# Attention with sinks, SoLU and routed experts on one core: the last products with v one step sooner, the next pair's first transposes one step later, and x rounded beside those transposes' copies

## The chip, the cores and the metric

The kernel runs on one core of one Trainium2 chip. The metric is the time of one execution on the device, in microseconds (us); lower is better.

## The reference

Three parts follow one another. Only the first is touched by the change.

```python
def _attn_ref(q, k, v, n_sink, window):          # 2 batches, 8 heads, 768 tokens, 64 wide
    scores = scale * np.matmul(q, k.transpose(0, 1, 3, 2))
    keep = is_sink | in_window                   # 4 sink columns, a window of 128
    scores = np.where(keep, scores, -1000000000.0)
    scores = scores - np.max(scores, axis=-1, keepdims=True)
    a = np.exp(scores)
    a = a / (np.sum(a, axis=-1, keepdims=True) + 1e-09)
    return np.matmul(a, v).astype(np.float32)

x = attn_out.transpose(0, 2, 1, 3).reshape(1536, 512)
x = _moe_ref(x)     # softmax-gated layer of 1024, layer norm, back to 512
out = _moe2_ref(x)  # 8 experts: relu(x @ w1[e]) @ w2[e], weighted by 8 rounds of row and column scaling
```

## The kernel before, in words

**Pairs and steps.** The 16 heads of the attention are worked off as 8 pairs (p = 0 to 7). The two heads of a pair lie on the upper and lower 64 rows of q, k and the output. A pair has 6 steps (t = 0 to 5), one for each tile of 128 queries; in each step there are two tiles of scores, one for each head, numbered k = 2t and 2t + 1. A tile is 128 x 128 (t = 0), 128 x 256 (t = 1) or 128 x 260 (the rest, where the four sink columns stand beside the window's 256).

**One program for each engine.** Each engine has its own list of instructions, written out by hand, and semaphores hold the lists together. In every step each engine first does the new tiles, and then calls a function `back(p, t)`, which holds the work that lags behind. The order in `back` is what the change edits, in three engines:

- TensorE: `scores(p, t + 1)` (L722), then in `back` the transposes of the probabilities (`turn(p, b)`, L742, b = 0, 1, 2 for the tiles t = 2b and 2b + 1), those of the sink columns (`turn_sinks`, L750), the products with v (`pv(p, b)`, L766), and those of the sinks (`pv_sinks`, L773), which complete the pair's x, a sum of 128 x 768 in PSUM. Most of a pair's `back` work is done while the next pair's scores are made.
- VectorE: `mask_max` (L1270, adds the mask, takes the row maximum, and empties a bank of scores; each of the two tiles of a step), then in `back` `normalise` (L1278, L1282, L1285: sum plus a small number, reciprocal, head 0's tile times it), `copy_pT` (L1291, copies head 1's transposes out of PSUM) and `rest_x` (L1303, x minus its rounded part, the low half of x).
- ScalarE: `exp_tile` (L1042, for each of the two tiles of a step), then in `back` `copy_pT` (L1049, head 0's transposes), `scale_probs` (L1057), `copy_sinkT` (L1061) and `round_x` (L1066, the rounded part of x).
- GpSimd multiplies head 1's tiles by the reciprocals (L517), splits sink columns (L540, L543), and splits the weights of the second part into a rounded and a remaining half (L556, L559, L565, L571), between these.

**What waits for what.** `rest_x(p)` waits for `round_x(p)`, and that for `pv_sinks(p)`. The first product of the next pair, `pv(p + 1, 0)`, writes into the same sum, so it waits for `rest_x(p)`. There are four banks for scores, so `scores` of a tile waits until the tile four before it has been through `mask_max`. Transposes use two banks in turn, so each waits until the use two before it has been copied. The ScalarE's `exp_tile(p, k)` waits for `mask_max(p, k)`; VectorE's `normalise(p, b)` waits for the four exponentials of its tiles.

**After the pairs** TensorE begins the second part (`h1_half`, L797 to L799) and does the last pair's remaining work between its halves.

Of the kernel before, what the change touches and what calls it, by code (L numbers as in the profile page):

```python
# [38 lines left out]
PAIRS = BATCH * HEADS // 2  # L39
# [21 lines left out]
def solu_moe(nc: bass.Bass, n_sink, window, qT, kT, v, w_in, w_out, g_ln, w_gate, w_exp, out):  # L61
# [5 lines left out]
    with ExitStack() as ctx:  # L67
# [75 lines left out]
        def x1(part, c, at, n):  # L143

            half, at = divmod(at, SEQ)
            at += half * 2 * HALF_X + part * HALF_X + c * SEQ
            return xw[:, at:at + n]
# [137 lines left out]
        def tile_probs(p, t, h):  # L285
            at = h * PW + k_from(t, h)
            return probs[:, p % 2, t, at:at + width(t)]
# [14 lines left out]
        def t_use(b, h):  # L302
            return 2 * b + h

        def t_bank(p, use):
            return bank(T_BANK + (T_USES * p + use) % 2)
# [5 lines left out]
        def copied(p, use):  # L312

            if use in ACT_USES:
                return pT_act, len(ACT_USES) * p + ACT_USES.index(use) + 1
            return pT_dve, len(DVE_USES) * p + DVE_USES.index(use) + 1

        def x_psum(t0, t1):
            return ps[:, XP + t0 * P:XP + t1 * P]
# [382 lines left out]
        def _(pe):  # L702
# [29 lines left out]
            def turn(p, b):  # L732

                for h in range(2):
                    use = t_use(b, h)
                    pe.wait_ge(probs_ready[h], BATCHES * p + b + 1)
                    if h == 0:
                        pe.wait_ge(probs_scaled, BATCHES * p + b + 1)
                    bank_free(p, use)
                    for n in range(T_FIRST[b], T_END[b]):  # L740
                        at = (n - T_FIRST[b]) * P
                        last = pe.transpose(t_bank(p, use)[:, at:at + P], p_block(p, h, n), ident[:, :])  # L742
                    last.then_inc(pT_full, 1)

            def turn_sinks(p):

                pe.wait_ge(sinks_split, p + 1)
                bank_free(p, SINK_USE)
                for t in range(2, QT):
                    last = pe.transpose(t_bank(p, SINK_USE)[0:SINK_ROWS, (t - 2) * P:(t - 1) * P],  # L750
                                        sink_cols[:, t - 2, :].bitcast(F32), ident[:, :])
                last.then_inc(pT_full, 1)

            def pv(p, b):

                for h in range(2):
                    pe.wait_ge(*copied(p, t_use(b, h)))
                if b == 0:
                    pe.wait_ge(v_loaded[p % 2], 128 * (p // 2 + 1))
                    if p > 0:  # L760
                        pe.wait_ge(x_out, p)
                for j, t0, t1 in (((0, 0, 2), (1, 1, 2)), ((1, 2, 3), (2, 2, 4)),
                                  ((3, 3, 5), (4, 4, 6), (5, 5, 6)))[b]:
                    n = j + t0
                    for h in range(2):
                        pe.matmul(x_psum(t0, t1)[64 * h:64 * h + 64, :], v_sb[:, p % 2, h, j * DH:(j + 1) * DH],  # L766
                                  pT[:, h, n * P:(n + t1 - t0) * P],
                                  start=(j, t0) in ((0, 0), (1, 2)), stop=False, skip_group_check=True)

            def pv_sinks(p):  # L770
                pe.wait_ge(*copied(p, SINK_USE))
                pe.wait_ge(v_sinks_split, p + 1)
                pe.matmul(x_psum(2, QT), v_sink_r[:, p % 2, :], sinkT[:, :],  # L773
                          start=False, stop=True, skip_group_check=True).then_inc(x_full, 1)

            def back(p, t):

                if t == 0 and p > 0:
                    turn(p - 1, 1)
                if t == 1 and p > 0:  # L780
                    pv(p - 1, 0)
                if t == 2 and p > 0:
                    turn(p - 1, 2)
                if t == 3 and p > 0:
                    turn_sinks(p - 1)
                    pv(p - 1, 1)
                if t == 4:
                    if p == 0:
                        pe.wait_ge(consts, 3)
                    turn(p, 0)  # L790
                if t == 5 and p > 0:
                    pv(p - 1, 2)
                    pv_sinks(p - 1)

            def three(o, ws, xs, first, last):

# [24 lines left out]
            for p in range(PAIRS):  # L821
                for t in range(QT):
# [4 lines left out]
                    back(p, t)  # L827
            h1_half(0, 0)
            back(PAIRS, 0)
            h1_half(0, 1)  # L830
            back(PAIRS, 1)
# [1 line left out]
            back(PAIRS, 2)  # L833
            h1_half(1, 1)
            back(PAIRS, 3)
            back(PAIRS, 5)


            def turn_ln(b, f):
# [195 lines left out]
        def _(act):  # L1035
# [9 lines left out]
            def copy_pT(p, b, h):  # L1045
                use = t_use(b, h)
                n0, n1 = T_FIRST[b], T_END[b]
                act.wait_ge(pT_full, T_USES * p + use + 1)
                act.activation(pT[:, h, n0 * P:n1 * P], t_bank(p, use)[:, 0:(n1 - n0) * P],  # L1049
                               ACT.Copy).then_inc(pT_act, 1)  # L1050

            def scale_probs(p, b):

                act.wait_ge(norm_link, 2 * (BATCHES * p + b + 1))
                a = tile_probs(p, 2 * b + 1, 0)
                k = 4 * b + 2
                act.activation(a, a, ACT.Copy, scale=a_stat[:, A_INV, k:k + 1]).then_inc(probs_scaled, 1)  # L1057

            def copy_sinkT(p):
                act.wait_ge(pT_full, T_USES * p + SINK_USE + 1)  # L1060
                act.activation(sinkT[:, :], t_bank(p, SINK_USE)[0:SINK_ROWS, 0:(QT - 2) * P],  # L1061
                               ACT.Copy).then_inc(pT_act, 1)

            def round_x(p):
                act.wait_ge(x_full, p + 1)
                act.activation(x1(0, p % DC, p // DC * SEQ, SEQ), x_psum(0, QT), ACT.Copy).then_inc(x_hi_out, 1)  # L1066

            def back(p, t):

                if t == 0 and p > 1:  # L1070
                    round_x(p - 2)
                if t == 0 and p > 0:
                    copy_pT(p - 1, 1, 0)
                    scale_probs(p - 1, 2)
                if t == 2:
                    if p > 0:
                        copy_pT(p - 1, 2, 0)
                    scale_probs(p, 0)
                if t == 3 and p > 0:
                    copy_sinkT(p - 1)  # L1080
                if t == 4:
                    copy_pT(p, 0, 0)
                    scale_probs(p, 1)

            for p in range(PAIRS):
                for t in range(QT):
# [175 lines left out]
        def _(dve):  # L1262
# [11 lines left out]
            def normalise(p, b):  # L1274

                s = slice(4 * b, 4 * b + 4)
                dve.wait_ge(exp_done, STEPS * p + 4 * b + 4)
                dve.tensor_scalar(a_stat[:, A_DEN, s], a_stat[:, A_SUM, s], EPS, None,  # L1278
                                  ALU.add).then_inc(norm_link, 1)
                n = 2 * (BATCHES * p + b)  # L1280
                dve.wait_ge(norm_link, n + 1)
                dve.reciprocal(a_stat[:, A_INV, s], a_stat[:, A_DEN, s]).then_inc(norm_link, 1)  # L1282
                dve.wait_ge(norm_link, n + 2)
                a = tile_probs(p, 2 * b, 0)
                dve.tensor_scalar(a, a, a_stat[:, A_INV, 4 * b:4 * b + 1], None, ALU.mult).then_inc(probs_ready[0], 1)  # L1285

            def copy_pT(p, b, h):
                use = t_use(b, h)
                n0, n1 = T_FIRST[b], T_END[b]
                dve.wait_ge(pT_full, T_USES * p + use + 1)  # L1290
                dve.tensor_copy(pT[:, h, n0 * P:n1 * P],  # L1291
                                t_bank(p, use)[:, 0:(n1 - n0) * P]).then_inc(pT_dve, 1)
# [7 lines left out]
            def rest_x(p):  # L1300
                dve.wait_ge(x_hi_out, p + 1)
                c, at = p % DC, p // DC * SEQ
                dve.tensor_tensor(x1(1, c, at, SEQ), x_psum(0, QT), x1(0, c, at, SEQ).bitcast(F32),  # L1303
                                  ALU.subtract).then_inc(x_out, 1)

            def back(p, t):

                if t == 0 and p > 0:
                    normalise(p - 1, 2)
                    if p > 1:  # L1310
                        rest_x(p - 2)
                    copy_pT(p - 1, 1, 1)
                if t == 2:
                    normalise(p, 0)
                    if p > 0:
                        copy_pT(p - 1, 2, 1)
                if t == 3 and p > 0:
                    rest_v_sinks(p - 1)
                if t == 4:
                    normalise(p, 1)  # L1320
                    copy_pT(p, 0, 1)


# [280 lines left out]
```

## Time and profile before

| | |
|---|---|
| median of three runs | 1254.23 us (1253.05 to 1255.44) |
| the profiled execution's own time | 1253.09 us |
| its span, first to last instruction | 1251.3 us |
| granted TensorE clock | 1.00 of full speed throughout |
| busy over the span | TensorE 99%, VectorE 55%, ScalarE 29%, GpSimd 43% |
| attention, up to the first product of the second part | the first 93.9 us |

The shares are means over stages with different limits. From 100 us on TensorE has no gaps; the attention is the only stage where it is not always busy. In the profile's rows L12 is a line of the kernel; "[0.62 <-DVE xw L1303]" behind an instruction says that its engine stood idle for 0.62 us before it, and that the wait was ended by VectorE's instruction of line 1303. PE is TensorE, DVE is VectorE, ACT is ScalarE, POOL is GpSimd.

### The profile page before, as it was taken

What the parts mean: (1) busy time and instruction counts of PE and PEld (TensorE: products, weight loads), DVE (VectorE), ACT (ScalarE), POOL (GpSimd) and SP (SyncE); (2) the same over time, 40 slices, a digit from 0 to 9 for tenths busy, and PEclk for the clock granted to TensorE, in tenths of its full rate; (3) what the DMA queues carried; (4) which work ended last, traced back from release to release, by engine and by line L of the source; (5) the groups of instructions that cost most, each with busy time, mean ns of one, the idle gap of its engine ahead of it and who ended that gap; (6) DMA issues with size and microseconds to landing.
All of it is one profiled execution on the core that took longest, in us unless ns stands there. A gap on an engine that the chain in (4) does not pass through costs nothing.

```text
span 1251.3 us, 18785 instructions
## 1 busy us (share of the span) xinstructions
PE 1236.2 (99%) x6446; PEld 1097.3 (88%) x6446; DVE 691.7 (55%) x1348; ACT 365.1 (29%) x832; POOL 535.7 (43%) x625
## 2 busy tenths in 40 slices
PE   7999999999999999999999999999999999999998
PEld 4558899989988999999999999999999999999997
DVE  7895734356665555555555555555555555555554
ACT  7884634312233222222222222222222222222221
POOL 7772315644444444444444444444444444444440
PEclk9999999999999999999999999999999999999999
DMA  6440000111110111111111111111111111111102
GB/s 204 156 149 18 1 1 1 34 35 34 34 35 28 38 36 36 34 34 34 34 34 34 34 34 34 34 34 34 34 34 34 34 34 34 34 34 34 35 18 101
DMA packets 57264, 53.13 MB, mean 42 GB/s; under 512 B 4352, under 2 KB 44544, under 8 KB 57216
## 3 DMA queue, kind: packets, MB, share of 16 engines
q1 hardware_dynamic: 56928, 52.19, 13.1%
q8 instruction: 27, 0.44, 0.1%
q10 hardware_dynamic: 288, 0.33, 0.1%
q14 instruction: 21, 0.17, 0.0%
HBM read 49.35 MB, written 3.15 MB: 42 GB/s over the span
## 4 chain that ended last, share of the span: by engine, by line
PE 95%; ACT 2%; DVE 2%; DMA 1%; issue 1%; SPq 0%; DVEq 0%; ACTq 0%
PE ps L797 30%; PE ps L798 30%; PE ps L799 30%; PE ps L722 2%; PE ps L766 1%; PE ps L742 1%; PE ps L847 1%; ACT probs L1042 1%; ACT acc L1218 1%; DVE probs L1270 1%; DMA k_sb<-kT 0%; PE ps L977 0%; DVE xw L1303 0%; ACT xw L1066 0%; DMA q_sb<-qT 0%
## 5 line engine op out<-in xcount | busy, mean ns | idle before, releaser
L1528 DVE SCALAR_TENSOR_TENSOR acc<-ps,gate_now,acc 128x512 f32<-128x512 f32 x336 | 252.1, 750 | 166.2 <-PE ps L799 162.0
L797 PE MATMUL ps<-ring 128*128 128x512 f32 x768 | 300.6, 391 | 0.0
L798 PE MATMUL ps<-ring 128*128 128x512 f32 x768 | 299.8, 390 | 0.0
L799 PE MATMUL ps<-ring 128*128 128x512 f32 x768 | 299.2, 390 | 0.0
L1200 ACT ACTIVATE sums<-ps 128x384 f32<-128x384 f32 x192 | 94.4, 492 | 597.8 <-PE ps L799 597.8
L1504 DVE TENSOR_TENSOR sums<-ps,sums 128x384 f32<-128x384 f32 x192 | 106.9, 557 | 158.2 <-ACT sums L1200 106.9
L799 PEld LDWEIGHTS ps<-ring 128*128 128x128 f32 x768 | 144.3, 188 | 30.9
L797 PEld LDWEIGHTS ps<-ring 128*128 128x128 f32 x768 | 144.2, 188 | 27.9 <-DVE acc L1524 0.4
L798 PEld LDWEIGHTS ps<-ring 128*128 128x128 f32 x768 | 144.2, 188 | 25.8
L642 POOL TENSOR_TENSOR w_raw<-w_raw 128x256 f32<-128x256 f32 x32 | 23.7, 741 | 321.3 <-PE ps L799 321.3
L797 PE MATMUL ps<-xw,ring 128*128 128x384 f32 x448 | 152.5, 340 | 0.3 <-ACT sums L1200 0.2
L1510 DVE SCALAR_TENSOR_TENSOR ring<-sums,ring 128x384 fp32r<-128x384 f32 x192 | 112.0, 583 | 72.9 <-ACT ring L1211 72.9
L799 PE MATMUL ps<-xw,ring 128*128 128x384 f32 x448 | 151.0, 337 | 0.0
L798 PE MATMUL ps<-xw,ring 128*128 128x384 f32 x448 | 150.9, 337 | 0.0
L797 PE MATMUL ps<-xw,w_b 128*128 128x384 f32 x448 | 150.5, 336 | 0.0
L799 PE MATMUL ps<-xw,w_b 128*128 128x384 f32 x448 | 150.3, 336 | 0.0
L798 PE MATMUL ps<-xw,w_b 128*128 128x384 f32 x448 | 150.0, 335 | 0.0
L671 POOL TENSOR_SCALAR ring<-w_in 128x1024 fp32r<-128x1024 f32 x32 | 33.8, 1056 | 233.0 <-PE ps L799 178.2
L1211 ACT ACTIVATE ring<-sums 128x384 fp32r<-128x384 f32 x192 | 100.1, 521 | 85.7 <-DVE sums L1504 85.7
L797 PEld LDWEIGHTS ps<-xw,ring 128*128 128x128 f32 x448 | 84.1, 188 | 2.6 <-ACT sums L1200 0.5
L798 PEld LDWEIGHTS ps<-xw,w_b 128*128 128x128 f32 x448 | 84.3, 188 | 2.0
L797 PEld LDWEIGHTS ps<-xw,w_b 128*128 128x128 f32 x448 | 84.1, 188 | 1.9
(148 smaller groups left out, 1765.2 us busy)
## 6 DMA issues: line engine op xcount, KB each, us to landing
w_in<-w_exp SPq DMA_DIRECT2D x64, 256.0 KB, 3.2
w_raw<-w_exp SPq DMA_DIRECT2D x64, 128.0 KB, 2.8
w_raw<-w_exp SPq DMA_DIRECT2D x32, 256.0 KB, 3.2
v_sb<-v SPq DMA_DIRECT2D x16, 192.0 KB
out<-acc SPq DMA_DIRECT2D x12, 256.0 KB, 2.0
q_sb<-qT SPq DMA_DIRECT2D x7, 384.0 KB, 4.4
k_sb<-kT SPq DMA_DIRECT2D x7, 384.0 KB, 4.9
k_sb<-kT SPq DMA_DIRECT2D x9, 256.0 KB, 5.7
```

What stands on the lines that cost most here:

```text
L642: pool.tensor_tensor(raw(4), raw(0), raw(3), ALU.add).then_inc(w1_sums, 1)
L671: pool.tensor_scalar(w2c(0, 0, 2 * BANK), w2_raw(0, 2 * BANK), 1.0, 0.0, ALU.mult, ALU.add).then_inc(w2_hi, 1)
L722: pe.matmul(bank(k % S_BANKS)[:, 0:w], q_sb[rows_h, p % 2, t * P:(t + 1) * P], k_sb[rows_h, p % 2, k_at(t), at:at + w], start=True, stop=T ...
L742: last = pe.transpose(t_bank(p, use)[:, at:at + P], p_block(p, h, n), ident[:, :])
L797: pe.matmul(o, ws[0], xs[0], start=first, stop=False, skip_group_check=True)
L798: pe.matmul(o, ws[0], xs[1], start=False, stop=False, skip_group_check=True)
L799: return pe.matmul(o, ws[1], xs[0], start=False, stop=last, skip_group_check=True)
L1200: act.activation(part_sum(m, s), a_bank(s), ACT.Copy).then_inc(part_copied, 1)
L1211: act.activation(h_at(0, i, b * BLK, BLK), a_bank(s) if m == C12 else c_sum(m), ACT.Relu).then_inc(h_hi_out, 1)
L1504: dve.tensor_tensor(c_sum(m), at, part_sum(part, s), ALU.add).then_inc(c_summed, 1)
L1510: dve.scalar_tensor_tensor(out=h_at(1, i, b * BLK, BLK), in0=a_bank(s) if m == C12 else c_sum(m), scalar=0.0, in1=h_at(0, i, b * BLK, BLK) ...
L1528: dve.scalar_tensor_tensor(out=acc[:, T, :], in0=y_bank(u, T), scalar=gate_now[:, T:T + 1], in1=acc[:, T, :], op0=ALU.mult, op1=ALU.add).t ...
```

## The change

In the steps t = 4 and t = 5 of a pair p, some lagging work changes places. On TensorE the last products of pair p - 1 with v and those of its sinks move from step 5 to step 4, and the first transposes of pair p from step 4 to step 5. The two copies of these transposes (ScalarE's and VectorE's) move from step 4 to step 5 too. `round_x` and `rest_x` of pair p - 1 move from step 0 of pair p + 1 to step 5 of pair p, and stand in front of these copies. After the last pair, TensorE's last call becomes `back(PAIRS, 4)`, which does what `back(PAIRS, 5)` did. Nothing is added and nothing is removed.

```diff
@@ TensorE, back(p, t)
-                if t == 4:
+                if t == 4 and p > 0:
+                    pv(p - 1, 2)
+                    pv_sinks(p - 1)
+                if t == 5:
                     if p == 0:
                         pe.wait_ge(consts, 3)
                     turn(p, 0)
-                if t == 5 and p > 0:
-                    pv(p - 1, 2)
-                    pv_sinks(p - 1)
@@ TensorE, after the pairs
-            back(PAIRS, 5)
+            back(PAIRS, 4)
@@ ScalarE, back(p, t)
-                if t == 0 and p > 1:
-                    round_x(p - 2)
                 if t == 0 and p > 0:
                     copy_pT(p - 1, 1, 0)
                     scale_probs(p - 1, 2)
...
                 if t == 4:
+                    scale_probs(p, 1)
+                if t == 5:
+                    if p > 0:
+                        round_x(p - 1)
                     copy_pT(p, 0, 0)
-                    scale_probs(p, 1)
@@ VectorE, back(p, t)
                 if t == 0 and p > 0:
                     normalise(p - 1, 2)
-                    if p > 1:
-                        rest_x(p - 2)
                     copy_pT(p - 1, 1, 1)
...
                 if t == 4:
                     normalise(p, 1)
+                if t == 5:
+                    if p > 0:
+                        rest_x(p - 1)
                     copy_pT(p, 0, 1)
```

On VectorE, from the two tiles of step 5 of a middle pair to the first tile of step 1 of the next, this stands in a row before (the `ISA` rows are `mask_max`, each with a second small row that reads its maximum; the last one here is the first tile of step 1):

```order
219 L1291 COPY pT<-ps 128x384 [waits pT_full]
220 L1270 ISA probs,a_stat<-ps,mask 128x260 [waits scores_full]
222 L1270 ISA probs,a_stat<-ps,mask 128x260 [waits scores_full]
224 L1270 ISA probs,a_stat<-ps,mask 128x128 [waits scores_full]
226 L1270 ISA probs,a_stat<-ps,mask 128x128 [waits scores_full]
228 L1278 TENSOR_SCALAR a_stat<-a_stat 128x4 [waits exp_done]
229 L1282 RECIPROCAL a_stat<-a_stat 128x4 [waits norm_link]
230 L1285 TENSOR_SCALAR probs<-probs,a_stat 128x260 [waits norm_link]
231 L1303 TENSOR_TENSOR xw<-ps,xw 128x768 [waits x_hi_out]
232 L1291 COPY pT<-ps 128x512 [waits pT_full]
233 L1270 ISA probs,a_stat<-ps,mask 128x256 [waits scores_full]
```

And this is the same stretch of the changed kernel, whose lines in this part are numbered one higher:

```order
219 L1271 ISA probs,a_stat<-ps,mask 128x260 [waits scores_full]
221 L1271 ISA probs,a_stat<-ps,mask 128x260 [waits scores_full]
223 L1304 TENSOR_TENSOR xw<-ps,xw 128x768 [waits x_hi_out]
224 L1292 COPY pT<-ps 128x384 [waits pT_full]
225 L1271 ISA probs,a_stat<-ps,mask 128x128 [waits scores_full]
227 L1271 ISA probs,a_stat<-ps,mask 128x128 [waits scores_full]
229 L1279 TENSOR_SCALAR a_stat<-a_stat 128x4 [waits exp_done]
230 L1283 RECIPROCAL a_stat<-a_stat 128x4 [waits norm_link]
231 L1286 TENSOR_SCALAR probs<-probs,a_stat 128x260 [waits norm_link]
232 L1292 COPY pT<-ps 128x512 [waits pT_full]
233 L1271 ISA probs,a_stat<-ps,mask 128x256 [waits scores_full]
```

The subtraction for x (128x768) has moved from behind the normalising to just behind the two tiles of step 5, and the copy of 384 columns from before these tiles to behind the subtraction.

On ScalarE, from step 4 of a middle pair to step 0 of the next, before (each `x2` is the two exponentials of a step):

```order
79 L1042 ACTIVATE probs,a_stat<-probs,a_stat 128x260 [waits scores_read] x2
80 L1049 ACTIVATE pT<-ps 128x384 [waits pT_full]
81 L1057 ACTIVATE probs<-probs,a_stat 128x260 [waits norm_link]
82 L1042 ACTIVATE probs,a_stat<-probs,a_stat 128x260 [waits scores_read] x2
83 L1042 ACTIVATE probs,a_stat<-probs,a_stat 128x128 [waits scores_read] x2
84 L1066 ACTIVATE xw<-ps 128x768 [waits x_full]
85 L1049 ACTIVATE pT<-ps 128x512 [waits pT_full]
```

The same stretch of the changed kernel:

```order
79 L1042 ACTIVATE probs,a_stat<-probs,a_stat 128x260 [waits scores_read] x2
80 L1057 ACTIVATE probs<-probs,a_stat 128x260 [waits norm_link]
81 L1042 ACTIVATE probs,a_stat<-probs,a_stat 128x260 [waits scores_read] x2
82 L1066 ACTIVATE xw<-ps 128x768 [waits x_full]
83 L1049 ACTIVATE pT<-ps 128x384 [waits pT_full]
84 L1042 ACTIVATE probs,a_stat<-probs,a_stat 128x128 [waits scores_read] x2
85 L1049 ACTIVATE pT<-ps 128x512 [waits pT_full]
```

The rounding of x now stands behind two exponentials of step 5, where it stood behind these and two more of step 0.

## Rows read from the trace of the kernel before

**Rows 1.** Busy time by stretch: three pairs, each from `mask_max(p, 2)` to the next, and a later stretch. Columns: length, then busy us (instructions) of PE, PEld, DVE, ACT, POOL, then clock, DMA.

```profile
28.35:40.24 11.89, 10.75 (x83) 6.82 (x81) 10.65 (x39) 10.09 (x34) 8.77 (x19) 1.00 0.56 182
40.24:51.62 11.38, 10.76 (x83) 6.76 (x81) 10.08 (x39) 9.75 (x32) 8.46 (x17) 1.00 0.54 173
...
63.01:74.74 11.73, 10.76 (x83) 6.76 (x81) 10.71 (x39) 9.87 (x32) 8.50 (x17) 1.00 0.52 182
...
100.00:150.00 50.00, 50.00 (x260) 40.67 (x259) 30.98 (x61) 25.91 (x45) 13.67 (x21) 1.00 0.00 1
```

**Rows 2.** Who waited for whom, 20 to 112 us: total us, times, longest.

```profile
PE ps L766 <- DVE xw L1303: 4.0, 5, 1.1
...
DVE xw L1303 <- ACT xw L1066: 1.4, 5, 0.5
```

**Rows 3.** The chain that ended last, one pair's turn: start us, us, what.

```profile
58.93 1.87 ACT probs L1042 x8
60.80 0.70 ACT xw L1066
61.53 0.97 DVE xw L1303
```

**Rows 4.** Timeline of DVE between two pairs: start us, us, instruction, idle before.

```profile
58.01 0.54 DVE L1291 COPY pT<-ps 128x384 f32<-128x384 f32 x1
58.48 0.41 DVE L1270 CUSTOM_DVE_ANT_0 probs<-ps,mask 128x260 f32<-128x260 f32 x1
...
59.17 0.28 DVE L1270 CUSTOM_DVE_ANT_0 probs<-ps,mask 128x128 f32<-128x128 f32 x1
...
60.06 0.17 DVE L1278 TENSOR_SCALAR a_stat<-a_stat 128x4 f32<-128x4 f32 x1 [0.40 <-ACT probs L1042]
...
61.53 0.96 DVE L1303 TENSOR_TENSOR xw<-ps,xw 128x768 fp32r<-128x768 f32 x1 [0.23 <-ACT xw L1066]
62.41 0.68 DVE L1291 COPY pT<-ps 128x512 f32<-128x512 f32 x1
63.01 0.41 DVE L1270 CUSTOM_DVE_ANT_0 probs<-ps,mask 128x256 f32<-128x256 f32 x1
```

**Rows 5.** Timeline of ACT in the same place.

```profile
59.44 0.50 ACT L1042 ACTIVATE probs<-probs,a_stat 128x260 f32<-128x260 f32 x1
...
59.94 0.39 ACT L1042 ACTIVATE probs<-probs,a_stat 128x128 f32<-128x128 f32 x1
...
60.70 0.80 ACT L1066 ACTIVATE xw<-ps 128x768 fp32r<-128x768 f32 x1
```

**Rows 6.** Timeline of PE around the moved work.

```profile
56.76 0.87 PE L742 MATMUL ps<-ident,probs 128*128 128x128 f32 x6
57.57 0.49 PE L722 MATMUL ps<-k_sb,q_sb 64*128 64x128 f32 x4
...
59.22 0.50 PE L773 MATMUL ps<-sinkT,v_sink_r 72*128 72x512 f32 x1
...
62.64 0.87 PE L766 MATMUL ps<-pT,v_sb 128*64 128x256 f32 x8 [0.62 <-DVE xw L1303]
```

**Rows 7.** Timelines of the second pair's end: PE at the load of q and k, DVE, POOL.

```profile
23.72 0.49 PE L722 MATMUL ps<-k_sb,q_sb 64*128 64x128 f32 x4 [1.27 <-DMA k_sb<-kT]
...
24.84 1.06 DVE L1278 TENSOR_SCALAR a_stat<-a_stat 128x4 f32<-128x4 f32 x1
...
24.59 1.28 POOL L571 TENSOR_TENSOR w_end<-w_raw,w_end 128x512 fp32r<-128x512 f32 x1
```

**Rows 8.** Timelines: one DVE operation of three pairs, and POOL's beside the longest.

```profile
20.14 0.28 DVE L1297 TENSOR_TENSOR v_sink_r<-v_sink,v_sink_r 8x128 fp32r<-8x128 f32 x1
...
55.62 0.50 DVE L1297 TENSOR_TENSOR v_sink_r<-v_sink,v_sink_r 8x128 fp32r<-8x128 f32 x1
...
67.00 0.86 DVE L1297 TENSOR_TENSOR v_sink_r<-v_sink,v_sink_r 8x128 fp32r<-8x128 f32 x1
...
66.45 1.27 POOL L565 TENSOR_TENSOR xw<-w_raw,xw 128x512 fp32r<-128x512 f32 x1
```

## The prediction, made before the changed kernel was run

> **What bounds the kernel now.** I read the busy times by stretch first. From 100 us on TensorE is busy for the whole of the stretch [rows 1]; the change touches nothing there, so a microsecond won or lost before it is one at the end. In the attention a pair takes 11.38 us (one in the middle 11.73, the first full one 11.89), with TensorE busy for 10.76, VectorE for 10.08 and ScalarE for 9.75 [rows 1]. No engine is full, and three are nearly so: a loop through several engines sets the pace. The list of waits names it: TensorE's first products with v wait for VectorE's subtraction for x (`rest_x`), 4.0 us in 5 times, and that one for ScalarE's rounding (`round_x`), 1.4 us in 5 times [rows 2]. The chain of waits goes through the same place in each pair: four exponentials, `round_x`, `rest_x` [rows 3], and then the product with v [rows 6].
>
> The reader is to see in VectorE's timeline how little room it has there. From the first tile of step 5 (58.48) to the first tile of step 1 (63.01) are 4.53 us, and it stands idle in them for only 0.40 (for the exponentials) and 0.23 (for `round_x`) [rows 4]. So its own work there is 4.53 - 0.63 = 3.90 us. TensorE waits 0.62 us in the same place [rows 6], as does ScalarE elsewhere: both follow VectorE.
>
> **The change part by part.** Nothing is added, so everything is a matter of who stands where.
>
> *TensorE.* Six transposes (0.81 us from start to start of what follows, 56.76 to 57.57) go behind the twelve products and the sinks' one; x of a pair is then complete one `turn` and one `scores` sooner. Before, the sinks' product starts at 59.22 [rows 6]; without the transposes (0.81) and the scores of the next pair's first tiles (0.4 of their 0.49, since instructions overlap) ahead of it, it starts near 58.0 and x is complete near 58.5. That is before ScalarE can come to it, as the next part shows, so x itself is never what is late.
>
> *ScalarE.* `round_x` now stands behind the two exponentials of step 5. The first starts 0.45 us behind its tile's `mask_max` (58.48 to 58.93), the second 0.51 later (59.44), and what follows 0.50 after that (59.94) [rows 3 to 5]: `round_x` can start 0.45 + 0.51 + 0.50 = 1.46 us after the first tile of step 5. Before, it stood two exponentials of step 0 later, at 60.70, which is 2.22 after.
>
> *VectorE.* `rest_x` starts 0.83 us after `round_x` starts (60.70 to 61.53) [rows 4, 5]: so 1.46 + 0.83 = 2.29 us after the first tile. But VectorE, which formerly had two more tiles and the normalising to do in between, now comes to it right after its two tiles, 0.69 us after the first one (58.48 to 59.17), with a last read of about 0.1. It stands idle for 2.29 - 0.69 - 0.1 = 1.5 us, in every pair. What it gets back: the 0.40 it waited for the exponentials (they are done long before, now) and the 0.23 for `round_x`. The copy of 384 columns (0.47, 58.01 to 58.48) moves from one side of this to the other: the stretch has it more, the rest of the pair has it less.
>
> Sum for a pair: +1.50 - 0.40 - 0.23 = **+0.87 us**. The stretch of 4.53 becomes 3.90 + 0.47 + 1.50 = 5.87, the rest of the pair (11.38 - 4.53 = 6.85) becomes 6.38, together 12.25.
>
> Is the idle time hidden by anything? What is queued behind `rest_x` on VectorE is the copy of the first transposes, then the tiles of step 0 of the next pair, then the normalising that GpSimd and ScalarE wait for. TensorE's next transposes wait for that copy (the bank rule), and the scores of step 2 wait for the tiles of step 0. TensorE has 0.62 us of idle time and no more to lend, and needs its turn with VectorE again within the pair. Nothing hides it.
>
> *The ends.* It counts from pair 2 on. The scores of pair 2 are held by the load of k until 23.72 [rows 7] in both orders. Before, VectorE is then stopped in a small operation of `normalise` for 1.06 us, until GpSimd's operation beside it ends (24.59 + 1.28 = 25.87; 24.84 + 1.06 = 25.90) [rows 7], and reaches the first tile of step 1 at 28.35 [rows 1]. After, the thirteen products stand ahead of the held scores, so x is complete before 23.72. I put `round_x` at 23.4 and `rest_x` 0.83 later, near 24.2 (an estimate); then 0.88 for it, 0.47 for the copy, 0.5 for two tiles of 128 (59.17 to 60.06, less 0.40), 1.24 for the normalising (60.06 to 61.53, less 0.23) and 0.60 for a copy [rows 4] bring the first tile of step 1 to about 27.9. The small operation now comes after 25.87 and isn't stopped: a gain of 0.5 us. From there five pair turns follow before the second part begins (three of them are in [rows 1]), and each costs 0.87. The last pair's idle time lies beside the first products of the second part and costs nothing.
>
> Sum: -0.5 + 5 x 0.87 = **+3.8 us**. Against the profiled execution (1253.09 us, 1.8 more than its span) this makes 1256.9; the median of the runs is 1.1 us above that execution, so against it 1254.2 + 3.8 = **1258.0 us**, +0.3%. About 0.2%, 2.5 us, is what a measurement of this kernel can tell from no change.
>
> **A price that is not in the sum: GpSimd.** The operation of 1.06 us [rows 7] and the one of 0.86 against 0.50 in another pair (67.00 + 0.86 = 67.86, right after GpSimd's 66.45 + 1.27 = 67.72) [rows 8] show VectorE's operations on SBUF ending just after one of GpSimd's. The slower of these pairs is the one of 11.73 instead of 11.38 [rows 1], so such a stop passes into the pair's time in full. The change moves VectorE's normalising against GpSimd's row of work: `normalise(p, 2)` comes about 1.2 us nearer to `normalise(p + 1, 0)`, so GpSimd's later work is still under way when VectorE comes to its next small operations. From below a pair gains 0.22 (0.50 down to 0.28 [rows 8]); from above it loses 0.36 (0.86 against 0.50), or more if two such operations meet one of GpSimd's. I take nothing, and keep -0.2 to +0.5 a pair for the range.
>
> The Trainium skill, "SBUF — State Buffer", section "Who interferes with whom", says that VectorE and GpSimd share a pair of ports as an exclusive lock, and whichever operation comes second is blocked until the first ends. By that rule, and these rows agree (the end at 25.90 behind 25.87), the order of arrival in the new rhythm decides, and the sum would be up to 2.5 us more.
>
> **The rivals.**
>
> 1. *TensorE sets the pace, and the change frees it.* x is complete sooner, `rest_x` is over long before the next pair's first product, and the wait of 0.62 (in all 4.0 us [rows 2]) goes, with nothing in its place. For it: this wait is the longest of TensorE's, and TensorE is the busiest of the three. Time: 1254.2 - 4.0 = 1250 us. It is decided by whether VectorE can spare 1.5 us in a pair: it would need idle time elsewhere of at least 0.9 us, and outside the stretch its timeline shows only 11.38 - 10.08 - 0.63 = 0.67, most of it gaps between dependent small operations. I give it 0.09.
> 2. *The gaps are shared out.* VectorE waits the 1.5 us, but the work after it is no longer held up by other waits and stops: GpSimd's stops fall away (-0.2), other waits (0.3 or so) too. Then a pair costs 0.3 to 0.4 and the total is -0.5 + 5 x 0.35 = +1.3: 1255.5 us. 0.15.
> 3. *GpSimd's stops get worse*: up to 0.5 a pair on top, +3.8 + 2.5 = +6.3: 1260.5 us. 0.16.
> 4. The forecast, +2.6 to +5.2: 0.60.
>
> **How the numbers follow.** The time is that of case 4. It alone spans 1256.8 to 1259.4. The range for 8 in 10 takes in most of cases 2 and 3 and leaves out case 1: 1255.4 to 1260.5. Slower by over 0.2%: case 4 and case 3, 0.76; within 0.2%: case 2 and what noise takes from the others, 0.15; faster: case 1, 0.09.
>
> **What would show it.** In the changed kernel: `rest_x` with an idle time before it near 1.5 us, released by `round_x`, in pairs 2 to 7; the wait of TensorE's first products for `rest_x` gone, and in its place waits of transposes on VectorE's copy and of scores on `mask_max`; pairs of about 12.2 us from one first tile of step 1 to the next; the second part beginning near 97.5 instead of 93.9; stretches from 100 us on unchanged in length. It is wrong if ScalarE's `round_x` starts before the exponentials' row says it can, if VectorE proves to have room (pairs below 11.4), or if small operations of VectorE get long beside GpSimd's (pairs of 12.7 and more).

## The result, and the profile after

| | before | after |
|---|---|---|
| median | 1253.64 us (6 runs, 1252.11 to 1255.93) | 1258.40 us (6 runs, 1257.93 to 1260.63) |
| profiled execution, its span | 1253.09, 1251.3 us | 1258.81, 1257.0 us |
| ratio to before | | 1.0047, 95% interval 1.0037 to 1.0057 |

The changed kernel is slower by 0.47%, and the interval lies wholly above the 0.2% that count as no change. (The ratio of the two medians is 1.0038; 1.0047 is the recorded estimate from all the runs, which the interval belongs to.) The forecast was 1258.0 us, +3.8 us. The spans differ by 5.7 us, and so the forecast's sum was too small by nearly 2 us; the medians differ by 4.8.

First the busy times of the changed kernel, from one `mask_max(p, 2)` to the next as in [rows 1] (length, then busy us of PE, PEld, DVE, ACT, POOL), and a late stretch:

```profile
27.52:40.34 12.82, 11.24 (x85) 6.81 (x81) 10.92 (x40) 10.20 (x34) 8.46 (x16) 1.00 0.57 191
40.34:53.15 12.81, 10.94 (x83) 6.66 (x79) 10.91 (x40) 9.98 (x32) 8.45 (x16) 1.00 0.47 153
53.15:65.95 12.80, 10.95 (x83) 6.66 (x79) 10.90 (x40) 9.98 (x32) 8.84 (x18) 1.00 0.49 150
65.95:78.75 12.80, 10.94 (x83) 6.66 (x79) 10.90 (x39) 9.98 (x32) 8.46 (x16) 1.00 0.46 165
...
100.00:150.00 50.00, 50.00 (x261) 40.69 (x260) 29.60 (x57) 24.28 (x45) 14.25 (x25) 1.00 0.04 11
```

A pair now takes 12.81 us instead of 11.38. TensorE is still full in the late stretch, so nothing is won back there. VectorE is busy for 10.91 us in a pair instead of 10.08 with the same instructions: 0.83 us of busy time without more work.

Who waited for whom in the changed kernel, 20 to 112 us (us in total, times, longest):

```profile
DVE xw L1304 <- ACT xw L1066: 10.9, 7, 1.8
...
PE ps L742 <- ACT pT L1049: 5.3, 5, 1.1
...
PE ps L742 <- DVE pT L1292: 2.3, 5, 0.5
...
PE ps L722 <- DVE a_stat L1271: 1.7, 5, 0.3
```

Against [rows 2]: VectorE's wait for `round_x` has grown from 1.4 to 10.9 us. TensorE's wait for `rest_x` (4.0 us) is gone, and in its place it waits 9.3 us for copies of transposes and for `mask_max`. Its timeline has the three places:

```profile
50.13 0.63 PE L742 MATMUL ps<-ident,probs 128*128 128x128 f32 x4 [1.07 <-ACT pT L1049]
51.21 0.63 PE L742 MATMUL ps<-ident,probs 128*128 128x128 f32 x4 [0.45 <-DVE pT L1292]
...
53.61 1.05 PE L722 MATMUL ps<-k_sb,q_sb 64*128 64x260 f32 x4 [0.34 <-DVE a_stat L1271]
...
99.50 0.47 PE L797 MATMUL ps<-xw 128*128 128x512 f32 x1 [0.41 <-DVE a_stat L1271]
```

The last of these rows is the first product of the second part: 99.50 against 93.88 before, 5.6 us later. That is the whole difference of the spans. The chain that ended last goes through the same place, over the two exponentials and the rounding to `rest_x` (start us, us, what; [rows 3] have it before, with four exponentials where two are now; each counts twice, with its small read):

```profile
47.81 1.10 ACT probs L1042 x4
48.91 0.70 ACT xw L1066
...
49.64 0.04 DVE xw L1304
```

VectorE's timeline for the stretch of [rows 4], and on to the next first tile of step 5:

```profile
47.35 0.42 DVE L1271 CUSTOM_DVE_ANT_0 probs<-ps,mask 128x260 f32<-128x260 f32 x1
...
49.64 0.96 DVE L1304 TENSOR_TENSOR xw<-ps,xw 128x768 fp32r<-128x768 f32 x1 [1.51 <-ACT xw L1066]
50.51 0.55 DVE L1292 COPY pT<-ps 128x384 f32<-128x384 f32 x1
...
53.15 0.41 DVE L1271 CUSTOM_DVE_ANT_0 probs<-ps,mask 128x256 f32<-128x256 f32 x1
...
54.72 0.81 DVE L1279 TENSOR_SCALAR a_stat<-a_stat 128x4 f32<-128x4 f32 x1
...
57.39 0.89 DVE L1298 TENSOR_TENSOR v_sink_r<-v_sink,v_sink_r 8x128 fp32r<-8x128 f32 x1
...
60.16 0.41 DVE L1271 CUSTOM_DVE_ANT_0 probs<-ps,mask 128x260 f32<-128x260 f32 x1
```

The stretch from 47.35 to 53.15 has grown from 4.53 to 5.80 us: 0.47 for the copy that moved into it, and 0.80 of time lost. `rest_x` starts 2.29 us after the first tile, as forecast, with 1.51 us of idle time before it. The rest of the pair (53.15 to 60.16) is 7.01 us, where the forecast had 6.38. Two small operations are long in it, an addition of `normalise(p, 0)` of 0.81 us (such an addition takes 0.17 in [rows 4]) and the subtraction for the sinks' part of v (`rest_v_sinks`) of 0.89 (0.50 in [rows 8]). GpSimd's timeline beside them:

```profile
54.31 0.61 POOL L556 TENSOR_SCALAR xw<-w_raw 128x512 fp32r<-128x512 f32 x1
54.89 0.62 POOL L559 TENSOR_SCALAR w_end<-w_raw 128x512 fp32r<-128x512 f32 x1
...
56.86 1.27 POOL L565 TENSOR_TENSOR xw<-w_raw,xw 128x512 fp32r<-128x512 f32 x1
```

54.89 + 0.62 = 55.51, and VectorE's addition ends at 54.72 + 0.81 = 55.53. 56.86 + 1.27 = 58.13, and its subtraction ends at 57.39 + 0.89 = 58.28. The addition started while the first of GpSimd's two roundings ran, and was held through the second as well. In the kernel before, the same addition came when GpSimd's second rounding was all but over (52.64 + 0.61 = 53.25), and was not held; the copy behind it then waited for its transposes:

```profile
52.64 0.61 POOL L559 TENSOR_SCALAR w_end<-w_raw 128x512 fp32r<-128x512 f32 x1
...
53.21 0.17 DVE L1278 TENSOR_SCALAR a_stat<-a_stat 128x4 f32<-128x4 f32 x1
...
54.21 0.69 DVE L1291 COPY pT<-ps 128x512 f32<-128x512 f32 x1 [0.30 <-PE ps L742]
```

### The profile page after: what moved, and what is told of

The parts are those of the page before. It is cut to its first block, busy times and chain, and to the rows that moved or that the text cites. A ratio compares the mean times of both kernels' runs of the same rounds, so it can differ in the third digit from the quotient of the medians.

```text
span 1257.0 us, 18785 instructions
## 1 busy us (share of the span) xinstructions
PE 1237.0 (98%) x6446; PEld 1097.1 (87%) x6446; DVE 693.8 (55%) x1348; ACT 365.8 (29%) x832; POOL 535.7 (43%) x625
## 4 chain that ended last, share of the span: by engine, by line
PE 93%; DVE 2%; ACT 2%; issue 1%; DMA 1%; POOL 0%; SPq 0%; DVEq 0%; ACTq 0%
PE ps L797 30%; PE ps L798 30%; PE ps L799 30%; PE ps L722 1%; DVE probs L1271 1%; PE ps L742 1%; PE ps L847 1%; DMA k_sb<-kT 1%; ACT probs L1042 1%; ACT acc L1219 1%; PE ps L977 0%; DVE v_sink_r L1298 0%; DVE pT L1292 0%; ACT xw L1066 0%; PE ps L766 0%
```

## The experiments

Two questions are put. Is it the place of x's two halves that costs, by VectorE's wait for `round_x` (theory A), or TensorE's new order, by transposes that come too late to be copied (theory B)? And are GpSimd's stops a cost of their own? All kernels compute the reference's result in full. Ratios are to the kernel before, on the same chip; a pair is again the time from one `mask_max(p, 2)` to the next, read from each profile at the middle pairs.

| kernel | median us | before, same chip | ratio (95% interval) | pair us |
|---|---|---|---|---|
| changed, `rest_x` back | 1252.91 | 1253.01 | 0.9994 (0.9985 to 1.0003) | 11.63 |
| changed, both halves of x back | 1255.21 | 1253.01 | 1.0028 (1.0016 to 1.0039) | 12.01 |
| before, `round_x` early | 1252.31 | 1253.01 | 0.9993 (0.9984 to 1.0002) | 11.26 to 11.77 |
| changed, GpSimd's rounding later | 1257.43 | 1253.01 | 1.0033 (1.0021 to 1.0046) | 12.35 |
| changed, `round_x` first | 1250.92 | 1252.73 | 0.9986 (0.9977 to 0.9995) | 11.37 |
| the two above together | 1250.48 | 1252.73 | 0.9981 (0.9972 to 0.9990) | 11.25 |
| before, `round_x` early, v's subtraction later | 1248.80 | 1252.73 | 0.9968 (0.9956 to 0.9980) | 10.84 |
| changed, `round_x` first, v's subtraction later | 1250.32 | 1252.73 | 0.9980 (0.9971 to 0.9989) | 11.26 |
| before, v's subtraction later | 1251.02 | 1252.97 | 0.9987 (0.9978 to 0.9996) | 11.16 |
| changed, v's subtraction later | 1254.35 | 1252.97 | 1.0018 (1.0009 to 1.0027) | 12.20 |

### `rest_x` put back behind the normalising

```diff
@@ changed kernel, VectorE, back(p, t)
                     normalise(p - 1, 2)
+                    if p > 1:
+                        rest_x(p - 2)
                     copy_pT(p - 1, 1, 1)
...
                 if t == 5:
-                    if p > 0:
-                        rest_x(p - 1)
                     copy_pT(p, 0, 1)
```

> The changed kernel, with only the subtraction for x (rest_x) put back to where it stood, behind the normalising of step 0; round_x, the copies and TensorE's order stay as changed. Theory A (VectorE's 1.5 us of waiting for round_x sets the cost, and GpSimd's stops add to it): the wait of 1.5 us is gone, VectorE stops at most 0.35 us for TensorE's transposes instead, and a pair, 12.8 us in the changed kernel and 11.4 before, takes 11.4 to 11.8; the time is within 2.5 us of before. Theory B (the order on TensorE is what costs, since the transposes now end later than VectorE wants to copy them): VectorE waits 1 us and more for the transposes in the same place, a pair stays at 12 us or more, and the time is 3 us or more above before.

A pair fell from 12.81 to 11.63 us, and the time is that of the kernel before. That is what theory A expected. (GpSimd's two stops are gone here as well, so the 1.18 us that a pair fell by are not the wait alone.) VectorE's timeline shows that theory B names a real wait too:

```profile
60.32 0.56 DVE L1292 COPY pT<-ps 128x384 f32<-128x384 f32 x1 [0.98 <-PE ps L742]
```

From 25 to 84 us this wait is 0.89 to 0.98 us in five pairs and 0.57 in one. It was expected at 0.35 at most. With the transposes later on TensorE, VectorE comes to their copy early; that the changed kernel hides the same time under the wait for `round_x` is a reading here, and the run with `round_x` first bears it out. What is left of the change in this kernel, TensorE's new order with the early `round_x`, costs a pair 0.25 us (11.63 against 11.38), a sixth of the loss.

### Both halves of x put back

```diff
@@ changed kernel, with the edit above, ScalarE, back(p, t)
+                if t == 0 and p > 1:
+                    round_x(p - 2)
                 if t == 0 and p > 0:
                     copy_pT(p - 1, 1, 0)
...
                 if t == 5:
-                    if p > 0:
-                        round_x(p - 1)
                     copy_pT(p, 0, 0)
```

> The changed kernel with both parts of x (round_x on ScalarE, rest_x on VectorE) back in step 0; only TensorE's swap and the two copies stay as changed. Theory A: the wait of rest_x for round_x is 0.2 to 0.4 us again, a pair takes 11.4 to 11.9 us, the time is within 3 us of before. Theory B: pairs of 12 us or more, 3 us or more above before.

12.01 us a pair, just above theory A's 11.4 to 11.9 and at the edge of B's. The time does not choose between them either: the runs scatter from 1254.3 to 1260.7 us, and the excess over the kernel before is 2.2 us by the medians and 3.5 by the ratio, on either side of the 3 us. VectorE waits for the transposes and then for `round_x`, one after the other:

```profile
60.23 0.56 DVE L1292 COPY pT<-ps 128x384 f32<-128x384 f32 x1 [0.99 <-PE ps L742]
...
62.63 0.96 DVE L1304 TENSOR_TENSOR xw<-ps,xw 128x768 fp32r<-128x768 f32 x1 [0.28 <-ACT xw L1066]
```

TensorE's swap and its two copies therefore cost 0.63 us a pair, if nothing of x is moved with them. The expectation had both theories too far apart: what the swap costs depends on where x's halves stand.

### The kernel before with `round_x` at the end of step 5

```diff
@@ kernel before, ScalarE, back(p, t)
-                if t == 0 and p > 1:
-                    round_x(p - 2)
                 if t == 0 and p > 0:
                     copy_pT(p - 1, 1, 0)
...
                     copy_pT(p, 0, 0)
                     scale_probs(p, 1)
+                if t == 5 and p > 0:
+                    round_x(p - 1)
```

> The kernel before, with only round_x moved, to the end of step 5, where x has just been completed; rest_x stays behind the normalising of step 0. Theory A says that the loop exponentials, round_x, rest_x, tiles of the next pair holds the pair, and that VectorE's idle 0.23 us for round_x and TensorE's 0.62 us for rest_x can go once round_x is early: pairs of 11.0 to 11.2 instead of 11.4, the time 1 to 2 us below before. Rival: the two exponentials of step 0 come 0.7 us later and VectorE's or ScalarE's next waits take the place: no difference beyond 0.1%.

No difference that can be told. The wait of 0.23 us before `rest_x` is gone as expected, yet the pairs did not get shorter (11.72, 11.49, 11.26, 11.77 and 11.27 us). The reading is that the time went to GpSimd's stops: VectorE's small subtraction for v takes 0.71 us in one pair and 1.22 in the next, where it took 0.50 and 0.86. It is tried further down, by moving that subtraction.

```profile
55.78 0.71 DVE L1297 TENSOR_TENSOR v_sink_r<-v_sink,v_sink_r 8x128 fp32r<-8x128 f32 x1
...
61.59 0.94 DVE L1303 TENSOR_TENSOR xw<-ps,xw 128x768 fp32r<-128x768 f32 x1
...
67.05 1.22 DVE L1297 TENSOR_TENSOR v_sink_r<-v_sink,v_sink_r 8x128 fp32r<-8x128 f32 x1
```

### The changed kernel with GpSimd's rounding of weights behind the next normalising

```diff
@@ changed kernel, GpSimd
                 normalise(p, 0)
                 if p > 0:
+                    round_segments(p)
                     rest_w_in(p)
...
                 round_v_sinks(p)
-                if p + 1 < PAIRS:
-                    round_segments(p + 1)
```

> The changed kernel, with GpSimd's rounding of a pair's two pieces of weights (0.6 us each) moved behind the next pair's first normalising, so that it no longer runs while VectorE does the small addition of normalise(p, 0). If GpSimd's stop of 0.82 us of that addition is part of the cost: it takes 0.17 again, and a pair takes 0.3 to 0.4 us less than 12.8 (the rest of the 0.65 is covered by VectorE's former wait of 0.3 for the transposes), the time is 1.5 to 2.0 us below the changed kernel, some 3 us above before. If the stop is hidden elsewhere: pairs of 12.8 us and no difference to the changed kernel.

The stop is part of the cost: a pair takes 12.35 instead of 12.81. The addition takes 0.17 again, VectorE's subtraction for v 0.42, and a third small operation is now held (0.43; this kernel's lines are numbered one lower):

```profile
67.58 0.17 DVE L1278 TENSOR_SCALAR a_stat<-a_stat 128x4 f32<-128x4 f32 x1
...
68.59 0.69 DVE L1291 COPY pT<-ps 128x512 f32<-128x512 f32 x1 [0.30 <-PE ps L741]
...
70.00 0.42 DVE L1297 TENSOR_TENSOR v_sink_r<-v_sink,v_sink_r 8x128 fp32r<-8x128 f32 x1
...
71.16 0.43 DVE L1278 TENSOR_SCALAR a_stat<-a_stat 128x4 f32<-128x4 f32 x1
```

The rows add up to it: 0.25 (the copy of 128x512 starts 2.58 us after the first tile of step 1, where it started 2.83 after) + 0.47 (0.89 to 0.42) - 0.26 (0.17 to 0.43) = 0.46.

In all it gained less than five times 0.46, and less than the expectation had: the median is 4.4 us above the kernel before, where some 3 were expected, and the intervals of this run and of the changed kernel overlap. The first product of the second part starts at 98.19 instead of 99.50, since the second pair reaches its first tile of step 1 at 28.95 instead of 27.52. The cause of that lies in the trace: the moved work of GpSimd now meets VectorE's subtraction for v in the second pair, and holds it through three operations in a row (it took 0.30 us there in the changed kernel; 19.86 + 1.27 = 21.13, and 18.77 + 2.51 = 21.28).

```profile
18.77 2.51 DVE L1297 TENSOR_TENSOR v_sink_r<-v_sink,v_sink_r 8x128 fp32r<-8x128 f32 x1
...
19.86 1.27 POOL L565 TENSOR_TENSOR xw<-w_raw,xw 128x512 fp32r<-128x512 f32 x1
```

### The changed kernel with `round_x` ahead of step 5's exponentials

```diff
@@ changed kernel, ScalarE, back(p, t)
                 if t == 4:
                     scale_probs(p, 1)
+                    if p > 0:
+                        round_x(p - 1)
                 if t == 5:
-                    if p > 0:
-                        round_x(p - 1)
                     copy_pT(p, 0, 0)
```

> The changed kernel with one instruction moved on ScalarE: round_x stands ahead of step 5's two exponentials instead of behind them (x is complete some 0.6 us before ScalarE could start them). Everything else, TensorE's order and GpSimd's work with it, is as changed. Theory A (the 1.5 us that VectorE waits for round_x are the price): rest_x can start as soon as VectorE has done its two tiles, and it covers the wait for the transposes that showed (0.98 us) when rest_x was put back; the stretch from the first tile of step 5 to that of step 1 falls from 5.80 to 4.4 to 4.6 us, a pair takes 11.3 to 11.6 with GpSimd's stops as they are, and the time is 1 to 2 us below the kernel before. Rival: the exponentials, 0.7 us later, are what VectorE's next normalising waits for, and a pair stays at 12 us or more.

This is the run that decides. One instruction of ScalarE moved past two others, and the whole loss is gone: a pair takes 11.37 us, and the kernel is, if anything, faster than before (0.9986, interval up to 0.9995, which is less than the 0.2% that count as a change). VectorE's timeline:

```profile
57.12 0.96 DVE L1304 TENSOR_TENSOR xw<-ps,xw 128x768 fp32r<-128x768 f32 x1
58.00 0.55 DVE L1292 COPY pT<-ps 128x384 f32<-128x384 f32 x1
...
60.63 0.41 DVE L1271 CUSTOM_DVE_ANT_0 probs<-ps,mask 128x256 f32<-128x256 f32 x1
...
62.21 0.81 DVE L1279 TENSOR_SCALAR a_stat<-a_stat 128x4 f32<-128x4 f32 x1
...
64.87 0.89 DVE L1298 TENSOR_TENSOR v_sink_r<-v_sink,v_sink_r 8x128 fp32r<-8x128 f32 x1
```

No idle time stands before `rest_x` or the copy behind it, so `rest_x` covers the wait for the transposes. GpSimd's two stops are there in full, 0.81 and 0.89 us, as in the changed kernel. The wait of 1.51 us and the stops, which made the rest of the pair 0.63 longer, are thus separate terms, and this run takes away the first alone: 12.81 - 11.37 = 1.44.

### `round_x` first, with GpSimd's rounding later

The two edits above together.

> The kernel with round_x first and GpSimd's rounding of the weights behind the next pair's first normalising, both at once. If GpSimd's stops are a cost of their own that adds to the order of x, a pair takes 0.3 to 0.5 us less than with round_x first alone, 10.9 to 11.1, and the time is 3 us below before. If TensorE (10.4 us of work in a pair and a stagger of 0.35 in its scores) now sets the pace, no more than 0.1 us a pair is gained.

A miss: 11.25 us a pair, where 10.9 to 11.1 was expected, and no difference to `round_x` first alone that the intervals can tell. The stops are shorter (0.17, 0.42, 0.43; but in the second pair the subtraction is held for 2.50 us, as with GpSimd's rounding moved alone, and the pairs begin 2.06 us later than with `round_x` first alone). And x is now not complete in time. TensorE's sinks' product is what `round_x` waits for, and `rest_x` for it (the lines are again numbered one lower):

```profile
DVE xw L1303 <- ACT xw L1065: 2.5, 6, 0.5
ACT xw L1065 <- PE ps L772: 1.7, 6, 0.3
```

This is nearly the rival of that run, TensorE setting the pace (it is busy for 10.75 us of the pair by the trace, where the expectation took 10.4). The chain that ended last shows the loop, and neither VectorE nor GpSimd is in it from 60 to 74 us:

```profile
68.81 0.44 PE ps L772
...
69.28 0.82 ACT xw L1065
70.09 0.98 ACT probs L1041 x4
71.07 0.39 ACT pT L1048
...
71.60 1.07 PE ps L741 x8
```

From the sinks' product it goes through `round_x`, the two exponentials of step 5 and ScalarE's copy of the transposes, back to the transposes of TensorE that wait for that copy. Putting `round_x` ahead of the exponentials has taken it out of VectorE's way and left all three in TensorE's.

### `round_x` early in the kernel before, and the subtraction for v moved

```diff
@@ kernel before, with round_x at the end of step 5, VectorE, back(p, t)
-                if t == 3 and p > 0:
-                    rest_v_sinks(p - 1)
                 if t == 4:
+                    if p > 0:
+                        rest_v_sinks(p - 1)
                     normalise(p, 1)
```

> The kernel before, with round_x at the end of step 5 (as in the run that gained nothing) and VectorE's small subtraction for the sinks' v moved from step 3 to step 4, ahead of the normalising, where GpSimd was idle for 1.3 us. If GpSimd's stops of this operation (0.71 and 1.22 us instead of 0.28 in that run) took what the earlier round_x had given back, it takes 0.28 now and pairs of 10.9 to 11.1 appear, 1.5 to 2.5 us below before in all. If another loop holds the pair, it stays at 11.3 or more.

Pairs of 10.84 us (one of 10.95), the fastest kernel of the study: 0.9968 (0.9956 to 0.9980), 3.9 us below the median of before. Both are more than was expected (10.9 to 11.1, and 1.5 to 2.5 us). With the subtraction out of GpSimd's way the early `round_x` pays, which bears out the reading of the run that gained nothing. In front of the normalising GpSimd is idle, and the subtraction takes 0.28 us:

```profile
65.14 0.28 DVE L1297 TENSOR_TENSOR v_sink_r<-v_sink,v_sink_r 8x128 fp32r<-8x128 f32 x1
```

TensorE is now busy for 10.74 of a pair's 10.83 us (in the columns of [rows 1]), so waits and stops have next to nothing left to give:

```profile
60.45:71.28 10.83, 10.74 (x83) 6.75 (x80) 10.02 (x39) 9.81 (x32) 8.38 (x17) 1.00 0.58 200
```

### `round_x` first, and the subtraction for v moved

The same move in the kernel with `round_x` first.

> The kernel with round_x first, and the same move of VectorE's small subtraction for the sinks' v to step 4. It removes one of GpSimd's two stops (0.89 to 0.28 us) and leaves the other (the 0.82 us of the small addition): pairs 0.3 to 0.6 us shorter than with round_x first alone, the time 2 to 4 us below before. If stops are covered by waits, no difference to it.

A miss by size: 11.26 us a pair instead of 10.8 to 11.1. The subtraction takes 0.28, but 0.57 us of idle time before `rest_x` came back, released by `round_x`:

```profile
57.93 0.96 DVE L1304 TENSOR_TENSOR xw<-ps,xw 128x768 fp32r<-128x768 f32 x1 [0.57 <-ACT xw L1066]
```

The pair is that of `round_x` first with GpSimd's rounding later, and the chain that ended last has the same loop (55 to 70 us: sinks' product, `round_x`, exponentials, copy, transposes, without VectorE and GpSimd). That is why two different stops, each taken away from the kernel with `round_x` first, end at the same 11.25 us: in this order the loop is what is left.

### The subtraction for v moved alone, in both kernels

> The kernel before with only VectorE's small subtraction for the sinks' v moved from step 3 to step 4, ahead of the normalising; round_x stays in step 0. It tells the two moves of the fastest kernel apart (10.85 us a pair, with round_x early too; round_x alone gained nothing). If the two gains are independent, this one gives what GpSimd's stop cost, 0.22 us a pair (0.50 to 0.28) and 0.58 where it was 0.86, so pairs of 11.16 and 1.5 us less in all. If the loop through round_x holds the pair, it gives less, 0.1 or nothing, since the time won goes into VectorE's wait for round_x.

> The changed kernel with only the same move of VectorE's small subtraction. GpSimd stops it for 0.61 us in each pair of the changed kernel (0.89 instead of 0.28), and VectorE is without slack from there to the tiles of step 5: a pair falls from 12.81 to 12.2, the time by 2.5 to 3 us against the changed kernel, to about 2.5 to 3 us above before. If other waits take it up, less than half of that.

Both as expected by the pair: 11.16 us in the kernel before, and 12.20 in the changed one. So in the fastest kernel, taken in this order, 0.22 us a pair are GpSimd's stop and 0.32 the early `round_x`, which gained nothing by itself. In the changed kernel the stop of the subtraction cost the full 0.61 us. There the whole time fell to 1.4 us above before, where 2.5 to 3 were expected, and by more than five times 0.61, because the second pair ended 0.75 us sooner as well (first tile of step 1 at 26.77 instead of 27.52).

## Why the prediction was right, point by point

**The place was right.** The forecast said that VectorE would stand idle 2.29 - 0.69 - 0.1 = 1.5 us before `rest_x`; it is 1.51, and `rest_x` starts 2.29 us after the first tile of step 5. The stretch was to be 5.87 us and is 5.80. That this wait costs what it seems to is shown by the run with `round_x` first, where it alone is taken away, and a pair falls by 1.44.

**What hides nothing.** TensorE's waits moved from `rest_x` to VectorE's copy and `mask_max`, as forecast. The largest went to ScalarE's copy (1.07 us), which stands behind `round_x` too and which the forecast did not name.

**The term that was mis-sized is GpSimd's.** The forecast took nothing for it and kept -0.2 to +0.5 a pair. It measured +0.63, outside that range: the rest of the pair is 7.01 us against 6.38 forecast. By the rows, the addition's stop costs 0.24: it takes 0.64 longer, but VectorE's wait of 0.30 for the transposes behind it, which the run with GpSimd's rounding later shows again, is gone (and 0.1 of gaps), and the copy starts 2.83 us after the first tile of step 1 instead of 2.59. The subtraction's costs 0.37: the next tile starts 0.91 us after it, where it started 0.54 after. The step that failed is "I take nothing". One of the prediction's own signs of being wrong came with it, small operations of VectorE that get long beside GpSimd's and "pairs of 12.7 and more": the pairs are 12.81 us, where 12.25 were forecast. The trace of before had the material, though not the rows that the prediction showed: GpSimd's second rounding of 0.61 us ends just behind the start of the addition there, and as the normalising of one pair comes 1.2 us nearer to that of the next, it lies across the addition.

**The ends.** The gain in the second pair was put at 0.5 and is 0.83 (28.35 to 27.52). The second part was to begin near 97.5 us and began at 99.50. Its first product waits 0.41 us for the last `mask_max`, which the forecast did not have. Of the five turns two were longer before than the 11.38 that was reckoned with, 11.89 and 11.73 [rows 1], and all are near 12.8 now. From the first tile of step 1 to the next, four turns took 74.74 - 28.35 = 46.39 us before and 51.23 after: +4.84, with the fifth (11.38 to 12.8) some +6.3. Less 0.83, and with the wait of 0.41, this is the 5.6 us that the first product of the second part is late, within 0.3.

**What was luck.** The place and the size of the wait were right by their working; that 1258.0 us came so near to 1258.40 was not. Pairs longer than forecast by 0.56 us would have added 2.8 us to the sum of 3.8, and two things that the forecast did not have took 1.2 of them back: the five turns before were in sum 0.9 us longer than five times 11.38, and the second pair gained 0.33 more. The median of before came out at 1253.64 with more runs, where the forecast started from 1254.2.

**The rivals.** TensorE did not set the pace (the pair grew), but the two runs that stayed at 11.25, held by its loop with ScalarE, show how near it is. Case 3, GpSimd's stops, was what pushed the result from the forecast towards the upper end. Case 2, in which other waits and stops would shrink, went the wrong way: the stops grew.

What stays open: why the pairs of the kernel before with `round_x` early range from 11.26 to 11.77 us was read from the stops (0.71 and 1.22 us in two of them) and was not tried pair by pair; and why the second pair's end came at 26.5 to 30.0 us was followed up only where GpSimd's rounding was moved (the subtraction of 2.51 us).

## What to carry to other kernels

When work is moved to the place where its input is complete, look at what stands ahead of it on the engine that does its first half, and at what the engine of the second half has left to do before it. Here the input was early enough and the first half stood two instructions too late, and a nearly full engine waited 1.5 us in every round; one instruction moved turned +0.5% into -0.1%. When a wait is gone, read the chain again before taking away the next one: here the pair was then held by a loop in which the next two candidates had no part. Where two engines are held by one another's small operations, read how long the same small operation takes in different rounds before pricing a shift at nothing.

## What the runs showed of the hardware

A VectorE operation of 128 x 4 numbers (0.17 us undisturbed) was held through two GpSimd operations in a row, not only to the end of the one that was running: it started at 54.72, inside the first (54.31 to 54.92), and ended at 55.53, just behind the second (54.89 to 55.51). The Trainium skill, "SBUF — State Buffer", section "Who interferes with whom", has the exclusive lock for which the second to come waits; these rows agree with the lock. Between GpSimd's two instructions, which the profile shows overlapping by 0.03 us, VectorE did not get in. This was so in each of the six turns from 29 us on (0.81 to 0.82 us), and in the run with GpSimd's rounding later a subtraction was held through three GpSimd operations (2.51 us). It is not so each time: in the same changed kernel an earlier addition started inside one rounding (12.42 to 13.04) and ended just behind it, at 13.06, although GpSimd's next operation followed without a gap.

```profile
12.56 0.50 DVE L1279 TENSOR_SCALAR a_stat<-a_stat 128x4 f32<-128x4 f32 x1
...
12.42 0.62 POOL L559 TENSOR_SCALAR w_end<-w_raw 128x512 fp32r<-128x512 f32 x1
13.00 1.28 POOL L565 TENSOR_TENSOR xw<-w_raw,xw 128x512 fp32r<-128x512 f32 x1
```

What decides whether VectorE gets in between two of GpSimd's operations no run here shows.
